# Attention: couplings in quarters spread over the steps, and unread products in TensorE's wait for the second solve

## Chip, core and metric

One core of a Trainium2 chip runs one program of three stages (attention, a Fourier mixer with a feed-forward, a gated spatial unit). The metric is the device time of one execution in microseconds; the engines are TensorE (PE), VectorE (DVE), ScalarE (ACT), GpSimd (POOL), and SyncE (SP), which issues the DMAs.

## What is computed

The change lies in the attention stage, a delta-rule recurrence over 768 tokens for 4 batches of 8 heads (32 heads in all) of width 48:

```python
k_n = k / (np.linalg.norm(k, axis=-1, keepdims=True) + 1e-06)
state = np.zeros((B, H, D, D))
for t in range(S):
    kt, vt, bt = (k_n[:, :, t], v[:, :, t], beta[:, :, t, None])
    y[:, :, t] = np.einsum('bhd,bhde->bhe', q[:, :, t], state)
    v_old = np.einsum('bhde,bhd->bhe', state, kt)
    state = state + bt[:, :, :, None] * np.einsum('bhd,bhe->bhde', kt, vt - v_old)
```

Its result is cast to `[4, 768, 384]` and goes through `_moe_ref` (FFT over tokens and channels, layer norm, two weight products) and `_moe2_ref`; neither is touched but for the counts that they wait for.

## The kernel before

**Tiles.** The tokens are cut into chunks of C = 64. A chunk of one head is solved as a triangular system: with the gram matrix of its keys, the inverse of a unit lower triangular 64x64 matrix is formed, and then the chunk is a handful of small products. There are G = 6 groups; a group holds U = 32 units on each half of the 128 partitions (a unit is a chunk of a head), and is worked off in N = 8 steps of PR = 4 units, so 48 steps. Step k has i = k // 8 (its group) and n = k % 8.

**The inverse.** Each 64x64 inverse is made from its two 32x32 diagonal blocks and a corner. VectorE inverts the diagonal blocks of a whole group at once, 62 dependent column operations (lines 619 and 623) between a transpose in (line 583, `g_lane`, from `g_diag`) and two out (line 630 `t_rows`, line 632 `t_cols`). This is the solve. The corner is -T2 G21 T1, in two rounds of 32-row products on TensorE, the couplings: `couple_w` (line 461, evicted to `w_sb`, line 353) and `couple_x` (line 474, evicted to `tt`, line 361). Before, each of them is done for half a group (HU = 16 units) at a time. `corners` (line 371) spreads `t_cols` over `tt` with two masks. For the last group VectorE, then free, does these evictions (`last_inverse`, lines 655, 661, 666).

**Ahead of the solve** stand `piece("g", g, p)` and `piece("a", g, p)`: a quarter (QU = 8 units) of a group's gram or score products (line 449), 64x64 products, the dense pieces. Gram pieces are made three groups ahead, score pieces one. The couplings and the pieces share two PSUM banks `ps_ga` by turns; `uses` is the list that fixes the order, `turn` the place in it, `ga_done` and `ga_out` count products and evictions. For group 0 the diagonal blocks are copied to `g_diag` by VectorE, ScalarE and GpSimd (lines 638, 380, 309) after all four pieces; for later groups SyncE moves them by DMA.

**A step** on TensorE, in this order: P (line 500, keys by state into `ps_r`), U (line 518, inverse by right-hand side into `ps_u`), for the step before last Y (lines 535 and 540) and S (line 553, state), then pieces and couplings of this step. ScalarE evicts in the same order, each engine waiting by counts, and ScalarE also takes the square root of group i+2's norms in step `ROOT_STEP[i]` (6, 5, 4, 4), which waits for `glane_ok`. In group i before: x of the first half in step 0, w of the second in step 1, x of the second in step 2, w of the next group's first half in step 7; score pieces in steps 2 to 5, gram pieces in 5, 6, 7 and 0.

**Other users.** GpSimd scales v (line 277) and masks scores (line 270), in time with VectorE's columns. SyncE issues loads by the step counts. In the last group the mixer's loads are put into the steps (`ahead`), and its first products behind steps 5 and 6 (line 1110). The mixer starts from the results of the last group's step 4 of `y_sb`.

Of the kernel before, what the change touches and what calls it, by code (L numbers as in the profile page):

```python
# [19 lines left out]
def attention(nc, sems, kq_g, k_g, v_g, beta_g, x_scr):  # L20
# [25 lines left out]
    WARM = 46  # L46
    assert U == 32 and PR == 4 and x_scr.shape[0] == NB
# [3 lines left out]
    uses += [("w", 0, 0), ("x", 0, 0)]  # L51
# [6 lines left out]

    for k in range(STEPS):
        i, n = k // N, k % N  # L60
        if i and n == 0:
            uses += [("x", i, 0)]
        if i and 2 <= n < 6 and i + 1 < G:
            uses += [("a", i + 1, n - 2)]
        if gram_at(i, n):
            uses += [("g",) + gram_at(i, n)]
        if n == 1:
            uses += [("w", i, 1)]
        if n == 2:
            uses += [("x", i, 1)]  # L70
        if n == N - 1 and i + 1 < G:
            uses += [("w", i + 1, 0)]
    turn = {use: m for m, use in enumerate(uses)}

    with ExitStack() as ctx:
# [91 lines left out]
        def coupling(m, rows):  # L167
            return ps_ga[m % 2][rows, 0:HU * H].rearrange("p (u c) -> p u c", c=H)
# [96 lines left out]
        def gpsimd(pool, tokens_clear):  # L265
# [42 lines left out]
            pool.wait_ge(ga_out, turn["g", 0, 3] + 1)  # L308
            pool.tensor_copy(g_diag[quarter(3)], gram_sb[0][quarter(3), 1]).then_inc(dg_pool, 1)
            pool.wait_ge(dg_pool, 1)  # L310
# [11 lines left out]
        def scalar(act):  # L322
# [26 lines left out]
            def solved_w(g, c):  # L349
                m = turn["w", g, c]  # L350
                us = slice(HU * c, HU * c + HU)
                act.wait_ge(ga_done, m + 1)
                act.activation(w_sb[:, us], coupling(m, slice(0, P)), ACT.Copy).then_inc(ga_out, 1)

            def solved_x(g, c):
                m = turn["x", g, c]
                us = slice(HU * c, HU * c + HU)
                act.wait_ge(ga_done, m + 1)
                act.wait_ge(corner_ok, 2 * g + c + 1)
# [4 lines left out]
            def corners(g, c):  # L364

                us = slice(HU * c, HU * c + HU)
# [22 lines left out]
            corners(0, 0)  # L389
            solved_x(0, 0)  # L390
            for k in range(STEPS + 2):
# [11 lines left out]
                if 0 < i < G - 1 and n == 0:  # L403
                    solved_x(i, 0)
# [15 lines left out]
                if i and 2 <= n < 6 and i + 1 < G:  # L420
                    piece("a", i + 1, n - 2)
                if gram_at(i, n):
                    piece("g", *gram_at(i, n))
                if i < G - 1 and n == 1:
                    solved_w(i, 1)
                    corners(i, 1)
                if i < G - 1 and n == 2:
                    solved_x(i, 1)
                if i + 2 < G and n == ROOT_STEP[i]:
                    roots(i + 2)  # L430
                if n == N - 1 and i + 1 < G - 1:
                    solved_w(i + 1, 0)
                    corners(i + 1, 0)

        def tensor(pe, ahead):
# [17 lines left out]
            def couple_w(g, c):  # L453
                m = turn["w", g, c]
# [10 lines left out]
            def couple_x(g, c):  # L465
                m = turn["x", g, c]
# [3 lines left out]
                for j in range(HU):  # L470
                    u = HU * c + j
# [12 lines left out]
            couple_x(0, 0)  # L484
            pe.wait_ge(ident_ok, 2)
            for k in range(STEPS + 2):
# [16 lines left out]
                if 1 <= k <= STEPS:  # L503
                    j0 = k - 1
                    g, m, c = j0 // N, j0 % N, (j0 // NB) % 2
# [15 lines left out]
                if 0 < i < G and n == 0:  # L521
                    couple_x(i, 0)
# [38 lines left out]
                if i and 2 <= n < 6 and i + 1 < G:  # L561
                    piece("a", i + 1, n - 2)
                if gram_at(i, n):
                    piece("g", *gram_at(i, n))
                if n == 1:
                    couple_w(i, 1)
                if n == 2:
                    couple_x(i, 1)
                if n == N - 1 and i + 1 < G:
                    couple_w(i + 1, 0)  # L570

        def vector(dve):
            NEWTON = 5

            def to_lanes(g):
# [3 lines left out]
                else:  # L579
                    dve.wait_ge(dg_dve, 2)  # L580
                    dve.wait_ge(dg_act, 1)
                    dve.wait_ge(dg_pool, 1)
# [43 lines left out]
            def unlanes(g):  # L626
                if g:
                    dve.wait_ge(ga_done, turn["x", g - 1, 1] + 1)
                    dve.wait_ge(corner_ok, 2 * g)
# [6 lines left out]
            dve.wait_ge(ga_out, turn["g", 0, 3] + 1)  # L636
            for a in (0, 2):
                dve.tensor_copy(g_diag[quarter(a)], gram_sb[0][quarter(a), 0]).then_inc(dg_dve, 1)
# [9 lines left out]
            def last_inverse(g):  # L648
# [3 lines left out]
                for c in range(2):  # L652
# [1327 lines left out]
```

## Time and profile before

| what | us |
|---|---|
| median of three runs | 887.49 (886.86 to 890.08) |
| profiled execution, its own time | 889.29 |
| its span, first to last instruction | 887.5 |
| PE busy | 822.8 (93%) |
| DVE busy | 473.3 (53%) |
| ACT busy | 294.3 (33%) |
| POOL busy | 197.8 (22%) |
| attention, up to the results that the mixer needs | 0 to 254.6 |

How to read it: busy shares are means over stages with different limits, so the attention part has to be read by itself. In the timeline and the chain of waits each line has the start, the length and what ran; brackets hold the idle time before it and what ended it; "issue" is time in which the engine waited for nothing that the profile shows. A product of f32 operands shows as two records, so a coupling batch of 32 products has x64.

### The profile page before, as it was taken

Reading aid. Unit: us, or ns where it says so; the run is one execution under the profiler, and the core shown is the slowest. Engines: PE = TensorE matmul, PEld = TensorE weight load, DVE = VectorE, ACT = ScalarE, POOL = GpSimd, SP = SyncE. Lnnn points to the kernel's source line nnn. Section 1 sums busy time; section 2 is a strip of 40 time slices with the busy share of each in tenths; the row PEclk is TensorE's granted clock in tenths of the full one; section 3 lists DMA queues with packets and bytes.
Section 4 is the critical chain, followed back from the end, with each engine's and each line's share of the span. In section 5 each row is a group of like instructions: output and inputs, shape, how many; then the busy total and the mean of one; then the engine's idle time right before and its main releaser. Section 6 shows DMA issues by size and latency. Waiting matters only on the chain.

```text
span 887.5 us, 24710 instructions
## 1 busy us (share of the span) xinstructions
PE 822.8 (93%) x10634; PEld 797.0 (90%) x10634; DVE 473.3 (53%) x1072; ACT 294.3 (33%) x656; POOL 197.8 (22%) x171
## 2 busy tenths in 40 slices
PE   7378999899886999999999999999999999999998
PEld 6377899888776999999999999999899899899898
DVE  4999999999278743443434443333732431431421
ACT  5235566656343121112211221122531431421412
POOL 2123123034005605300720000000222222222321
PEclk9658989889996999999999999999999999999999
DMA  6544445412572120111002003003410010000001
GB/s 196 147 132 125 139 131 155 118 57 80 164 248 96 59 68 18 53 51 40 18 18 71 0 18 119 18 18 112 144 54 31 23 53 35 18 0 36 19 1 54
DMA packets 38170, 65.14 MB, mean 73 GB/s; under 512 B 4345, under 2 KB 26178, under 8 KB 38082
## 3 DMA queue, kind: packets, MB, share of 16 engines
q1 hardware_dynamic: 38082, 63.85, 23.2%
q8 instruction: 69, 1.13, 0.5%
q14 instruction: 19, 0.16, 0.1%
HBM read 46.66 MB, written 14.16 MB: 69 GB/s over the span
## 4 chain that ended last, share of the span: by engine, by line
PE 62%; issue 21%; DVE 13%; POOL 2%; ACT 2%; DMA 1%; SPq 0%; POOLq 0%; DVEq 0%; ACTq 0%
PE m_ps_h L1189 12%; PE g_ps_v L1690 11%; PE m_ps_d L1174 11%; PE ps_ga L449 4%; PE g_ps_y L1690 3%; PE g_ps_u L1690 3%; DVE prod L619 3%; PE ps_r L500 3%; DVE t_lane L623 2%; PE ps_y L540 2%; PE ps_y L535 2%; PE ps_u L518 2%; PE ps_s L553 2%; POOL g_vn_lo L1587 2%; PE ps_ga L474 2%
## 5 line engine op out<-in xcount | busy, mean ns | idle before, releaser
L1374 DVE SCALAR_TENSOR_TENSOR m_h_lo<-m_ps_h,m_h_hi 128x512 fp32r<-128x512 f32 x72 | 49.7, 691 | 101.7 <-ACT m_h_hi L1051 101.7
L1174 PE MATMUL m_ps_d<-m_w_hi,m_h_hi 128*128 128x384 f32 x288 | 97.6, 339 | 0.0
L1174 PE MATMUL m_ps_d<-m_w_hi,m_h_lo 128*128 128x384 f32 x288 | 96.3, 335 | 0.0
L1174 PE MATMUL m_ps_d<-m_w_lo,m_h_hi 128*128 128x384 f32 x288 | 96.3, 334 | 0.0
L1051 ACT ACTIVATE m_h_hi<-m_ps_h 128x512 fp32r<-128x512 f32 x72 | 43.1, 598 | 151.7 <-PE m_ps_h L1189 151.5
L449 PE MATMUL ps_ga<-kq 64*64 64x64 f32 x1536 | 61.0, 236 | 19.0 <-DVE t_lane L623 12.4
L1189 PE MATMUL m_ps_h<-m_unt_hi,m_w_hi 128*128 128x256 f32 x432 | 75.3, 283 | 3.4 <-DVE m_h_lo L1374 2.4
L449 PEld LDWEIGHTS ps_ga<-kq 64*64 64x64 f32 x1536 | 57.3, 150 | 19.9 <-DVE t_lane L623 12.6
L1189 PE MATMUL m_ps_h<-m_unt_hi,m_w_lo 128*128 128x256 f32 x432 | 74.3, 281 | 0.0
L1189 PE MATMUL m_ps_h<-m_unt_lo,m_w_hi 128*128 128x256 f32 x432 | 74.2, 281 | 0.0
L619 DVE TENSOR_TENSOR prod<-g_lane,t_lane 128x31 f32<-128x31 f32 (+15 forms) x186 | 69.6, 374 | 6.2
L623 DVE TENSOR_TENSOR t_lane<-t_lane,prod 128x31 f32<-128x31 f32 (+15 forms) x186 | 66.3, 356 | 6.4
L1851 DVE TENSOR_TENSOR g_vs<-g_ps_v,g_bias 128x384 f32<-128x384 f32 x32 | 17.8, 558 | 92.3 <-PE g_ps_v L1690 92.0
L1587 POOL TENSOR_TENSOR g_vn_lo<-g_vn,g_vn_hi 128x512 fp32r<-128x512 f32 x24 | 30.6, 1288 | 161.3 <-ACT g_vn_hi L1629 161.3
L1189 PEld LDWEIGHTS m_ps_h<-m_unt_hi,m_w_hi 128*128 128x128 f32 x432 | 62.1, 191 | 4.2 <-DVE m_h_lo L1374 2.8
L1690 PE MATMUL g_ps_v<-g_ws_hi,g_vn_hi 128*128 128x384 f32 x192 | 64.4, 335 | 0.0
L1690 PE MATMUL g_ps_v<-g_ws_hi,g_vn_lo 128*128 128x384 f32 x192 | 64.2, 334 | 0.0
L1690 PE MATMUL g_ps_v<-g_ws_lo,g_vn_hi 128*128 128x384 f32 x192 | 64.1, 334 | 0.0
L1593 POOL TENSOR_TENSOR g_g<-g_vs,g_ut 128x384 f32<-128x384 f32 x32 | 36.7, 1147 | 113.9 <-DVE g_vs L1851 113.9
L1189 PEld LDWEIGHTS m_ps_h<-m_unt_hi,m_w_lo 128*128 128x128 f32 x432 | 61.4, 191 | 0.0
L1189 PEld LDWEIGHTS m_ps_h<-m_unt_lo,m_w_hi 128*128 128x128 f32 x432 | 61.4, 191 | 0.0
L540 PE MATMUL ps_y<-u_sb,score 64*64 64x48 f32 x768 | 56.2, 233 | 3.7 <-issue 3.5
(223 smaller groups left out, 1920.7 us busy)
## 6 DMA issues: line engine op xcount, KB each, us to landing
kq<-kq_g SPq DMA_DIRECT2D x48, 256.0 KB, 3.3
v_in<-v_g SPq DMA_DIRECT2D x12, 384.0 KB, 3.3
k_in<-k_g SPq DMA_DIRECT2D x12, 384.0 KB, 3.1
x_scr<-y_sb SPq DMA_DIRECT2D x24, 192.0 KB, 3.5
stage<-w_ch SPq DMA_DIRECT2D x6, 768.0 KB, 5.7
x_scr<-m_x_sb SPq DMA_DIRECT2D x24, 192.0 KB, 1.9
g_x<-x_scr SPq DMA_DIRECT2D x24, 192.0 KB, 4.5
out<-g_y SPq DMA_DIRECT2D x24, 192.0 KB, 1.9
```

The source lines that it names most:

```text
L449: last = pe.matmul(ps_ga[m % 2][lo:lo + C, C * j:C * j + C], x[:, 0], x[:, 0 if what == "g" else 1], start=True, stop=True)
L500: last = pe.matmul(ps_r[lo:lo + C, D * j:D * j + D], kq[i % 4][rows, 0, PR * n + j], s_sb[rows, b, j], start=False, stop=True, skip_group_ ...
L540: last = pe.matmul(ps_y[out, at:at + D], score[g % 2][rows, PR * m + j], u_sb[rows, j0 % 2, j], start=j0 < NB, stop=True)
L619: dve.tensor_tensor(x, g_lane[g % 2][:, j + 1:H, j].unsqueeze(2).broadcast_to([P, m, n]), t_lane[:, j, 0:n].unsqueeze(1).broadcast_to([P, ...
L623: dve.tensor_tensor(below, below, x, ALU.add).then_inc(chain, 1)
L1051: act.activation(h_hi[:, 2 * g:2 * g + 2], ps_h[g % 2][:, :].rearrange("p (f t) -> p f t", f=2), ACT.Relu).then_inc(h_hi_ok, 1)
L1174: last = pe.matmul(out, first[x], second[y], start=(k == 0 and m == 0), stop=(k == n - 1 and m == 2))
L1189: last = pe.matmul(ps_h[g % 2][:, C2 * (f % 2):C2 * (f % 2) + C2], w[:, d, P * f:P * f + P], t[:, d], start=(m == 0 and d == 0), stop=(m = ...
L1374: dve.scalar_tensor_tensor(h_lo[:, 2 * g:2 * g + 2].rearrange("p f t -> p (f t)"), ps_h[g % 2][:, :], 0.0, h_hi[:, 2 * g:2 * g + 2].rearra ...
L1587: pool.tensor_tensor(vn_lo[:, t], vn[:, t % 2], vn_hi[:, t].bitcast(F32), ALU.subtract).then_inc(vn_lo_ok, 1)
L1593: pool.tensor_tensor(g[:, n % 2], vs[:, n % 2], ut[:, f, HS * h:HS * h + HS], ALU.mult).then_inc(g_ok, 1)
L1690: last = pe.matmul(out, first[x], second[w], start=(k == 0 and m == 0), stop=(k == n - 1 and m == 2))
```

## The change

Couplings are done by quarters of a group (q = 0 to 3) and not by halves, and are placed by two functions: w 0 in step 7 of the group before, w 1, 2, 3 in steps 0, 1, 2, x 0 to 3 in steps 0, 2, 4, 6; in the last group earlier. Score pieces move from steps 2 to 5 to steps 1 to 4, so each step of groups 1 and 2 has one dense piece. `couple_x` takes its right operand from `tt` and waits for `corner_ok`, whose count goes from two to three a group. Before the couplings of group 1, TensorE does four products of 512 columns that nobody reads. The first diagonal is copied in three parts. The mixer's waits get the new counts. `ROOT_STEP` stays.

The pieces of the diff are, in order: the placing functions; the first diagonal on ScalarE (VectorE and GpSimd alike); the couplings on TensorE; the wait of the U products of step m; the couplings' places in a step, behind U and at the step's end (ScalarE evicts in the same places); and VectorE's order in the last group.

```diff
+    PARTS = ((1, 0, 16), (2, 16, 24), (3, 24, 32))
...
+    def score_at(i, n):
+        return (i + 1, n - 1) if 1 <= n < 5 and i and i + 1 < G else None
+    def w_at(i, n):
+        if n == N - 1:
+            return [(i + 1, 0)] if i + 1 < G else []
+        if i == G - 1:
+            return {0: [(i, 1)], 1: [(i, 2), (i, 3)]}.get(n, [])
+        return [(i, n + 1)] if n < 3 else []
+    def x_at(i, n):
+        if i == G - 1:
+            return {0: [(i, 0)], 1: [(i, 1)], 2: [(i, 2), (i, 3)]}.get(n, [])
+        return [(i, n // 2)] if n % 2 == 0 else []
...
+        def corner_count(g, q):
+            return 3 * g + min(q, 2) + 1
...
-            for p in range(4):
+            piece("g", 0, 0)
+            for p, u0, u1 in PARTS:
                 piece("g", 0, p)
-            act.wait_ge(ga_out, 4)
-            act.activation(g_diag[quarter(1)], gram_sb[0][quarter(1), 1], ACT.Copy).then_inc(dg_act, 1)
+                act.wait_ge(ga_out, turn["g", 0, p] + 1)
+                act.activation(g_diag[quarter(1), u0:u1], gram_sb[0][quarter(1), 1, u0:u1], ACT.Copy).then_inc(dg_act, 1)
...
+            def keep_warm(m):
+                x = kq[0][:, 0, 0:QU].rearrange("p u t -> p (u t)")
+                for _ in range(4):
+                    pe.matmul(ps_ga[m % 2][0:C, :], x[:, 0:C], x, start=True, stop=True)
+
+            def couple_w(g, q):
+                m = turn["w", g, q]
                 bank_free(m)
+                if (g, q) == (1, 0):
+                    keep_warm(m)
                 pe.wait_ge(trows_ok, g + 1)
-                for j in range(HU):
-                    u = HU * c + j
+                for j in range(QU):
+                    u = QU * q + j
...
+            def couple_x(g, q):
+                m = turn["x", g, q]
                 bank_free(m)
-                pe.wait_ge(tcols_ok, g + 1)
-                pe.wait_ge(ga_out, turn["w", g, c] + 1)
+                pe.wait_ge(corner_ok, corner_count(g, q))
+                pe.wait_ge(ga_out, turn["w", g, q] + 1)
...
-                        last = pe.matmul(coupling(m, upper)[:, j], w_sb[lower, u], t_cols[lower, u],
+                        last = pe.matmul(coupling(m, upper)[:, j], w_sb[lower, u], tt[g % 2][lower, u, H:C],
...
-                    if m % NB == 0:
-                        pe.wait_ge(corner_ok, 2 * g + c + 1)
-                        pe.wait_ge(ga_out, turn["x", g, c] + 1)
+                    if m % 2 == 0:
+                        pe.wait_ge(ga_out, turn["x", g, m // 2] + 1)
+                    if m == 0:
                         pe.wait_ge(v_ok, g + 1)
...
-                if 0 < i < G and n == 0:
-                    couple_x(i, 0)
+                if i < G:
+                    for x in x_at(i, n):
+                        couple_x(*x)
...
-                if i and 2 <= n < 6 and i + 1 < G:
-                    piece("a", i + 1, n - 2)
                 if gram_at(i, n):
                     piece("g", *gram_at(i, n))
-                if n == 1:
-                    couple_w(i, 1)
-                if n == 2:
-                    couple_x(i, 1)
-                if n == N - 1 and i + 1 < G:
-                    couple_w(i + 1, 0)
+                if score_at(i, n):
+                    piece("a", *score_at(i, n))
+                for w in w_at(i, n):
+                    couple_w(*w)
...
+                corners(slice(0, QU))
+                solved_w(0)
+                corners(slice(QU, 2 * QU))
+                corners(slice(2 * QU, U))
+                solved_x(0)
+                solved_w(1)
+                solved_x(1)
+                solved_w(2)
+                solved_w(3)
+                solved_x(2)
+                solved_x(3)
```

## Rows read from the trace of the kernel before

**Rows 1.** Page, part 2: TensorE's granted clock in 40 slices, tenths of full:
```profile
PEclk9658989889996999999999999999999999999999
```

**Rows 2.** TensorE's timeline near 80 us: start, us, instructions, idle before them:
```profile
81.51 1.92 PE L461 MATMUL ps_ga<-t_rows,gram_sb 32*32 32x32 f32 x64 [4.06 <-DVE t_rows L630]
```

**Rows 3.** Windows, groups 1 to 5: from:to, length, then PE, PEld, DVE, ACT, POOL:
```profile
81.50:119.22 37.72, 35.55 (x1153) 34.54 (x1153) 35.21 (x80) 22.30 (x58) 12.30 (x10) 0.87 0.43 123
119.22:155.76 36.54, 34.11 (x1155) 33.20 (x1153) 34.00 (x79) 23.29 (x59) 8.96 (x7) 0.91 0.49 140
155.76:191.73 35.97, 32.93 (x1058) 31.84 (x1056) 33.54 (x76) 21.51 (x55) 8.69 (x6) 0.86 0.34 94
191.73:225.49 33.76, 29.82 (x1028) 28.62 (x1025) 28.75 (x62) 20.76 (x54) 9.23 (x6) 0.95 0.28 81
225.49:254.60 29.11, 25.29 (x814) 23.88 (x813) 15.57 (x23) 11.83 (x36) 0.50 (x2) 0.94 0.62 195
```

**Rows 4.** VectorE's timeline: the transposes to t_rows of groups 1 to 5:
```profile
79.34 2.02 DVE L630 STREAM_TRANSPOSE t_rows<-t_lane 128x1024 f32<-128x1024 f32 x1
...
113.20 2.12 DVE L630 STREAM_TRANSPOSE t_rows<-t_lane 128x1024 f32<-128x1024 f32 x1
...
147.22 2.14 DVE L630 STREAM_TRANSPOSE t_rows<-t_lane 128x1024 f32<-128x1024 f32 x1
...
182.86 2.12 DVE L630 STREAM_TRANSPOSE t_rows<-t_lane 128x1024 f32<-128x1024 f32 x1
...
216.56 2.11 DVE L630 STREAM_TRANSPOSE t_rows<-t_lane 128x1024 f32<-128x1024 f32 x1
```

**Rows 5.** Windows along the granted clock, TensorE alone: from:to, length, busy, clock:
```profile
47.10:67.60 20.50, 17.71 (x437) 0.50 0.38 122
...
67.60:81.20 13.60, 9.64 (x325) 1.00 0.62 182
...
81.20:91.50 10.30, 9.99 (x250) 0.50 0.07 23
...
122.20:129.00 6.80, 6.80 (x166) 0.50 0.10 36
...
159.70:166.50 6.80, 6.15 (x135) 0.50 0.21 57
...
231.40:234.80 3.40, 3.40 (x76) 0.50 0.37 113
```

**Rows 6.** Chain of waits, 145 to 260 us: start, us, what:
```profile
168.19 1.13 PE ps_ga L461 x64
...
169.32 0.60 PE ps_r L500 x16
...
228.25 1.43 issue
...
250.60 0.83 PE m_ps_o L1110 x4
...
251.43 0.65 PE m_ps_e L1110 x4
```

**Rows 7.** Timelines of VectorE and ScalarE at the start:
```profile
11.67 2.13 DVE L638 COPY g_diag<-gram_sb 32x1024 f32<-32x1024 f32 x2 [9.65 <-ACT gram_sb L342]
...
13.85 1.28 ACT L335 ACT_TABLE_LOAD   x1
...
15.82 0.35 ACT L335 ACTIVATE root<-g_lane,tiny 128x32 f32<-128x32 f32 x1 [0.68 <-DVE g_lane L583]
```

**Rows 8.** Timelines of ScalarE and VectorE: square roots, and a transpose:
```profile
75.08 0.36 ACT L335 ACTIVATE root<-g_lane,tiny 128x32 f32<-128x32 f32 x1 [0.60 <-DVE g_lane L583]
...
140.92 2.00 DVE L583 STREAM_TRANSPOSE g_lane<-g_diag 128x1024 f32<-128x1024 f32 x1
...
144.77 0.34 ACT L335 ACTIVATE root<-g_lane,tiny 128x32 f32<-128x32 f32 x1
```

**Rows 9.** GpSimd's timeline: the scaling of v for group 4:
```profile
176.71 2.77 POOL L277 TENSOR_TENSOR v_in<-v_in,norm 128x1536 f32<-128x1536 f32 x1 [23.18 <-DMA v_in<-v_g]
```

More of the change, by code:

```diff
@@ L362, in solved_x, with corners @@
                 last.then_inc(ga_out, 1)
-            def corners(g, c):
-                us = slice(HU * c, HU * c + HU)
+            def corners(g, us):
                 act.wait_ge(tcols_ok, g + 1)
@@ L388, in scalar @@
             solved_w(0, 0)
-            corners(0, 0)
-            solved_x(0, 0)
+            corners(0, slice(0, QU))
             for k in range(STEPS + 2):
@@ L402, in scalar @@
                     preset(k + 1)
-                if 0 < i < G - 1 and n == 0:
-                    solved_x(i, 0)
+                if i < G - 1:
+                    for x in x_at(i, n):
+                        solved_x(*x)
                 if k >= 2:
@@ L419, in scalar @@
                     continue
-                if i and 2 <= n < 6 and i + 1 < G:
-                    piece("a", i + 1, n - 2)
                 if gram_at(i, n):
                     piece("g", *gram_at(i, n))
+                if score_at(i, n):
+                    piece("a", *score_at(i, n))
+                for g, q in w_at(i, n):
+                    if g < G - 1:
+                        solved_w(g, q)
                 if i < G - 1 and n == 1:
[L425 to L428, printed above, removed]
+                    corners(i, slice(QU, 2 * QU))
+                if i < G - 1 and n == 3:
+                    corners(i, slice(2 * QU, U))
                 if i + 2 < G and n == ROOT_STEP[i]:
@@ L431, in scalar @@
                 if n == N - 1 and i + 1 < G - 1:
-                    solved_w(i + 1, 0)
-                    corners(i + 1, 0)
+                    corners(i + 1, slice(0, QU))
         def tensor(pe, ahead):
@@ L635, in vector @@
                 dve.memset(t[:, :], 0.0).then_inc(s_zero, 1)
-            dve.wait_ge(ga_out, turn["g", 0, 3] + 1)
-            for a in (0, 2):
-                dve.tensor_copy(g_diag[quarter(a)], gram_sb[0][quarter(a), 0]).then_inc(dg_dve, 1)
+            for p, u0, u1 in PARTS:
+                dve.wait_ge(ga_out, turn["g", 0, p] + 1)
+                for a in (0, 2):
+                    dve.tensor_copy(g_diag[quarter(a), u0:u1], gram_sb[0][quarter(a), 0, u0:u1]).then_inc(dg_dve, 1)
             to_lanes(0)
@@ L651, in last_inverse, with corners @@
                 dve.wait_ge(u_done, N * (g - 1))
-                for c in range(2):
-                    us = slice(HU * c, HU * c + HU)
+                def corners(us):
                     for a in range(2):
@@ L657, in last_inverse, with solved_w, solved_x @@
                     part.then_inc(corner_ok, 1)
-                    m = turn["w", g, c]
+                def solved_w(q):
+                    m = turn["w", g, q]
                     dve.wait_ge(ga_done, m + 1)
                     dve.wait_ge(ga_out, m)
-                    dve.tensor_copy(w_sb[:, us], coupling(m, slice(0, P))).then_inc(ga_out, 1)
-                    m = turn["x", g, c]
+                    dve.tensor_copy(w_sb[:, QU * q:QU * q + QU], coupling(m, slice(0, P))).then_inc(ga_out, 1)
+                def solved_x(q):
+                    m = turn["x", g, q]
                     dve.wait_ge(ga_done, m + 1)
-                    dve.wait_ge(corner_ok, 2 * g + c + 1)
+                    dve.wait_ge(corner_ok, corner_count(g, q))
                     for a in (0, 2):
-                        part = dve.tensor_scalar(tt[g % 2][quarter(a), us, H:C], coupling(m, quarter(a)), -1.0, None,
-                                                 ALU.mult)
+                        part = dve.tensor_scalar(tt[g % 2][quarter(a), QU * q:QU * q + QU, H:C], coupling(m, quarter(a)),
+                                                 -1.0, None, ALU.mult)
                     part.then_inc(ga_out, 1)
+                corners(slice(0, QU))
[9 more added lines that the diff above has]
+                solved_x(3)
             last_inverse(G - 1)
         done = {"y_done": y_done, "s_done": s_done, "u_done": u_done, "y_ok": y_ok, "s_ok": s_ok, "states": STEPS - NB, "y_out": y_out, "ga_out": ga_out,
-                "ga_done": ga_done, "corner_ok": corner_ok, "pieces": len(uses), "steps": STEPS, "groups": G, "n": N}
+                "ga_done": ga_done, "corner_ok": corner_ok, "pieces": len(uses), "w_last": turn["w", G - 1, 3] + 1, "corners": 3 * G, "steps": STEPS, "groups": G, "n": N}
         return (sync, gpsimd, scalar, tensor, vector), done
@@ L1082, in scalar @@
             act.wait_ge(att["ga_done"], att["pieces"])
-            act.wait_ge(att["corner_ok"], 2 * last_group + 2)
+            act.wait_ge(att["corner_ok"], att["corners"])
             act.wait_ge(w_lo, DT - 1)
@@ L1254, in first_weights_split @@
                 dve.wait_ge(att["ga_done"], att["pieces"])
-                dve.wait_ge(att["corner_ok"], 2 * last_group + 2)
+                dve.wait_ge(att["corner_ok"], att["corners"])
                 for c in range(DT - 1):
```

66 lines of the change are left out of this document (28 added, 38 removed).

## The prediction

> **What bounds the kernel now.** First view: the granted clock in forty slices [rows 1]. It reads 8 or less in six of the first ten slices, which are the attention part, and 9 in all behind the thirteenth. Second: TensorE's wait for the second solve [rows 2]: its first coupling batch of group 1 starts at 81.51 after 4.06 us of idle that VectorE's t_rows ended. Until there VectorE sets the pace, and everything that shifts VectorE's start shifts 81.51. Third: TensorE's work by group [rows 3]. The five stretches start where the first coupling batch of groups 1 to 5 starts; the last ends at the y_sb on which the mixer waits. TensorE is busy 94, 93, 92, 88 and 87% of them, so it bounds this part. Fourth: when the solves end [rows 4]. t_rows is ready at 81.36, 115.32, 149.36, 184.98 and 218.67. TensorE asks for it at 81.51, 119.22, 155.76, 191.73 and 225.49: from the second on VectorE is 3.9, 6.4, 6.8 and 6.8 us ahead. That lead is all that a faster TensorE can win before VectorE bounds. Fifth: TensorE's clock [rows 5]. It stands at 0.50 (1.2 GHz) for 20.5 us from 47.1, for 10.3 from 81.2, for 6.8 from 122.2 and again from 159.7, and for 3.4 us each in three more stretches, of which the one at 231.4 stands for the others (in groups 3 and 4).
>
> **Price of the low clock.** A coupling batch of 64 takes 1.92 us at 1.2 GHz [rows 2] and 1.13 at 2.4 [rows 6]: factor 1.70. A busy microsecond at the low clock thus gives back 0.4. Busy time at the low clock [rows 5]: group 1, 10.0 (worth 4.0); group 2, 6.8 (2.7); group 3, 6.2 and 3.4 (3.8); groups 4 and 5, 3.4 each (1.4 each). Sum 13.3 us. Without it the groups would last 33.7, 33.8, 32.2, 32.4 and 27.7 us [rows 3].
>
> **Part 1, the first diagonal copied in three parts.** Before, VectorE starts two copies of 32x1024 only after the last gram piece, 2.13 us from 11.67; ScalarE loads its square-root table at 13.85 after copy and scores, and starts the root at 15.82, 0.68 after it was free, when the transpose ended [rows 7]. After, only the last quarter is left behind the last piece: VectorE 2.13/4, or about 0.6 with the fixed cost, so the transpose could start 1.3 us sooner. ScalarE then becomes the later one: of its copy a quarter is left, so its table is ready about 0.7 sooner, plus the 0.68 that it had to spare, less small waits between the parts. I take **0.9 us** (bounds 0.5 and 1.4) for root, chain and t_rows alike: the second solve ends at 80.46.
>
> **Part 2, group 0 under the second solve.** Its couplings start in quarters, so the first u step needs 0.96 us of products twice instead of 1.92 twice, and short evictions: about 1.6 us sooner, on top of the 0.9. This is not on the path. ScalarE's square root for group 2 stands in step 6, waits for VectorE's transpose already now (0.60 idle, root at 75.08 [rows 8]) and will do so 0.9 earlier. The last piece of group 0 then ends near 76.5 (before it ended at 81.51 - 4.06 = 77.45).
>
> **Part 3, the four unread products** (64 rows out, 512 columns, K of 128). No such row exists. Nearest: two products of 193 columns in 0.83 us, and the next two in 0.65 [rows 6]. By columns one of 512 costs 0.86 to 1.10, four 3.4 to 4.4 us; I take 3.9. They run from 76.5 to 80.4 against t_rows at 80.46: hidden, and at most 0.5 too long. Behind them in TensorE's queue stands the whole of group 1. What they bring is the clock: group 1 starts at 2.4 GHz, which is worth **4.0 us** (bounds 0 and 4.0).
>
> **Part 4, quarters and one dense piece to a step.** The number of coupling products stays, 4.5 us a group; a step loses either a second dense piece (step 5) or gets its missing one (step 1). TensorE's busy time is unchanged. Evictions are more and shorter (for x two of 32x256 instead of 32x512, with no drop in fixed cost, so some 0.4 us more of ScalarE a group): hidden, ScalarE is busy 22.30 of 37.72 us [rows 3]. x now waits for corner_ok instead of tcols_ok, that is, for a ScalarE eviction; it has the P products (0.60 us [rows 6]) and the U products, as many, as cover, about what w and corners of a quarter take. What is to be won is the clock of groups 2 to 5: all low stretches there begin in steps 0 to 2, where the full coupling batches (32-row products) stand beside a halt of about 1 us in instruction issue, as the 1.43 us at 228.25 [rows 6]. With half the couplings there and a dense piece in each step I expect most of the **9.3 us** to go; I keep one or two short stretches (bounds 0 and 9.3).
>
> **What is late next.** Two things cut the gain. (a) ScalarE's root for group i+2 keeps its place in step 4 or 5. In group 2 it ran at 144.77, behind a transpose that ended at 142.92 [rows 8]. Transpose minus 0.9 is 142.0; TensorE, 4.7 us ahead at the start (114.5 for 119.22) and 2.7 more without the low clock, would bring ScalarE there at 137.4. It stalls 4.6 us; TensorE can run one step further (about 1.8), so **2.8 us** are lost, and perhaps 1.4 with a clock that falls in this wait. (b) VectorE itself: t_rows 5 at 218.67 - 0.9 = 217.8; the interval before group 4 was 35.62 instead of 34 because GpSimd's v_in waited for its DMA until 176.71 [rows 9] and its 2.77 us then fell beside column steps; with loads issued sooner this 1.6 goes, so 216.15 is the **floor** for group 5.
>
> **The sum.** Group 1 starts at 80.6, ends at 114.3; group 2 may start at 114.5 (t_rows), 33.8 + 2.8 + 1.4 gives 152.5; + 32.2 = 184.7; + 32.4 = 217.1 for the start of group 5, before 225.49. In group 5 VectorE evicts: t_cols, corners of a quarter and w come 3 us after t_rows, so x starts near 219.2 and not at 218.9 (217.1 + 1.8 for the w products, P and U): + 0.3. Then 27.7: y_sb at 245.1 instead of 254.6, **9.5 us** saved. One short low stretch more in groups 3 to 5, 1.4 us: 8.1. The mixer's front is fed by that y_sb; its loads are tied to the same steps and shift along, nothing is added. The profiled execution has a span of 887.5 and a time of 889.29; 889.29 - 8.1 = 881.2. It lay 1.8 us over the median 887.49 of the three runs, which carries over: **879.5**.
>
> **Rivals.**
> A, the forecast: 0.65. Own range 875.5 (floor reached, no low stretch, 12 us) to 882.5.
> B, spreading doesn't hold the clock: the fall comes from a pause of the engine, not from what the products are. Then only the fall after the 4.06 us wait goes, 0.9 + 4.0 = 4.9 us, and 882.6 results; root and t_rows bind nowhere, since the lead is only 3.9 + 4.0. For it: the longest low stretch in the groups stands behind the only long wait. Against it: the stretch from 47.1 stays at 0.50 while TensorE is busy 17.7 of 20.5 us [rows 5], and the later falls have pauses of some 1 us, such as also stand in full-speed stretches. 0.20. The Trainium skill, "TensorE: Matmul & The Clock Gate", section "HAM oscillation — how this bites in real kernels", ties the fall to the engine's idle gaps between bursts; by that rule B is the outcome, and the busy but slow stretch from 47.1 speaks against it.
> C, the fill-in work doesn't carry the clock (it runs at 1.2 GHz and the rise comes later, or root's wait of group 0 lets it fall) and spreading helps little: 0.9 to 4 us, 883.5 to 886.6. 0.09.
> D, slower: the small couplings in steps 4 and 6 of group 0 keep it at 1.2 GHz up to the unread products. The last three steps (9.6 busy us in 13.6, now at 2.4 [rows 5]) then take 6.4 longer, the unread products up to twice 3.9 (less as the clock rises in them); from 77.45 - 2.5 that makes a start of group 1 near 88, 6.7 late, minus the 4.0 that its warm clock gives. With one low stretch more in each of four groups, 1.4 each, from the couplings in steps 4 and 6: +8.3, 895.8. It decides from the point where the unread products end later than 85.5. 0.06. Against it: the root of group 0 leaves TensorE time, and no start of group 1 is bound by it before.
>
> **How the numbers follow.** B's centre lies on the limit, so 0.6 of it counts as faster. Faster by over 0.5% (below 883.05; 0.5% is about what a measurement of this kernel can tell from no change): 0.65 + 0.13 = 0.78; same 0.17; slower 0.05. The range takes A and nearly all of B: 875.5 to 884.5.
>
> **What would show it.** Root of group 0 at 14.9. t_rows 1 near 80.5 and TensorE's wait before it about 0, with the clock at 1.00 until well behind 90. Four f32 products of 512 columns in 3.4 to 4.4 us. Clock near 1.00 in groups 2 to 5. In group 2 ScalarE waits for g_lane before the root. Group 5 starts at 216 to 218.5. Wrong would be: low stretches as before (B), unread products that end behind t_rows by microseconds (D), or an interval from group 5's start to y_sb over 31 us.

## The result and the profile after

The changed kernel takes 898.81 us (median; 895.77 to 902.07) where the kernel before takes 887.8 beside it: ratio 1.0121, 95% interval 1.0077 to 1.0164. It is slower by some 11 us, where 8 us of gain were forecast. The profiled execution has a span of 898.5 us and a time of 900.24, against 887.5 and 889.29 of before.

The granted clock in forty slices; [rows 1] answers to it. The slices about group 1 are now 9, and group 5 (the eleventh and twelfth) has fallen to 6 and 8:
```profile
PEclk9659999999686899999999999999999999999999
```

The windows of groups 1 to 5, columns as in [rows 3], which answer to them:
```profile
81.60:118.05 36.45, 32.94 (x1153) 31.22 (x1152) 33.94 (x80) 23.78 (x66) 10.90 (x9) 1.00 0.45 126
118.05:157.40 39.35, 32.91 (x1156) 31.25 (x1155) 36.50 (x88) 24.38 (x68) 9.04 (x7) 1.00 0.47 131
157.40:193.80 36.40, 32.10 (x1061) 30.31 (x1062) 33.84 (x76) 22.94 (x63) 8.72 (x6) 0.95 0.33 92
193.80:226.30 32.50, 29.34 (x1026) 27.56 (x1028) 25.31 (x52) 21.81 (x62) 9.12 (x6) 1.00 0.29 87
226.30:259.50 33.20, 32.13 (x813) 30.65 (x813) 15.32 (x31) 11.82 (x36) 0.50 (x2) 0.69 0.50 158
```
Read the third and the last but two columns together. In groups 1 to 4 the clock is 1.00, 1.00, 0.95, 1.00 where it was 0.87, 0.91, 0.86, 0.95, and TensorE is busy 5.1 us less in them. But the groups last 144.7 us where they lasted 144.0: the idle time, length minus busy, went from 11.6 to 17.4. Group 5 lasts 33.2 for 29.1 at a clock of 0.69.

The windows along the granted clock, TensorE alone, columns as in [rows 5]:
```profile
45.60:69.50 23.90, 20.70 (x469) 0.50 0.42 127
69.50:81.60 12.10, 11.89 (x300) 1.00 0.54 160
230.00:250.50 20.50, 20.43 (x476) 0.50 0.34 109
294.80:301.60 6.80, 5.53 (x26) 0.50 0.00 0
```

**The ledger.** From the start of group 1 to the y_sb that the mixer waits for, the length can be split in three: TensorE's busy time as it would be at 2.4 GHz (the busy time less 0.41 of what lay in stretches at 0.50; 0.41 is 1 - 1/1.70, the factor of the prediction), the price of the low clock (that 0.41), and idle time. This was done for all kernels, each by its windows. Column "G1, G2-5" is the time at 0.50 in group 1 and in groups 2 to 5. The mixer takes its batches in turns; a turn is counted from the start of the second piece of ScalarE's m_unt_hi (277.93 and 306.50 in before, 284.85 and 317.78 in after), and "front" goes from that y_sb to the second turn. Behind it, each of these executions took 580.7 to 581.0 us.

| kernel | couplings | full-speed work | low price | idle | length | at 0.50: G1, G2-5 | front |
|---|---|---|---|---|---|---|---|
| before | halves | 144.1 | 13.6 | 15.4 | 173.1 | 9.9, 23.9 | 51.9 |
| after | quarters | 149.7 | 9.8 | 18.5 | 177.9 | 0, 23.9 | 58.3 |
| e1, changed again | quarters | 148.5 | 11.2 | 16.3 | 175.9 | 3.4, 23.9 | 57.9 |
| e2 | halves | 144.0 | 10.5 | 14.5 | 169.0 | 0, 27.3 | 50.9 |
| e4 | quarters | 148.2 | 11.2 | 14.0 | 173.4 | 3.4, 23.9 | 57.6 |
| e5 | quarters | 147.9 | 13.9 | 14.7 | 176.4 | 3.4, 30.7 | 52.4 |
| e6 | halves | 144.4 | 13.4 | 16.8 | 174.7 | 9.2, 23.9 | 51.3 |
| e7 | quarters, last group halves | 148.8 | 10.7 | 15.4 | 175.0 | 3.4, 23.9 | 50.4 |
| e8 | halves | 143.4 | 13.9 | 15.8 | 173.1 | 3.4, 30.7 | 53.3 |
| e9 | quarters | 148.0 | 19.4 | 13.0 | 180.4 | 17.0, 30.7 | 57.4 |
| e10 | quarters | 148.6 | 16.7 | 15.8 | 181.1 | 6.8, 34.2 | 58.2 |
| e11 | halves | 143.4 | 13.6 | 15.5 | 172.5 | 3.4, 30.7 | 52.9 |

From before to after: work +5.6, low price -3.8, idle +3.1, start of group 1 +0.1, front +6.4. That is 11.4, and the spans differ by 11.0: 0.3 less lies behind the second turn, the rest is rounding. Each row is one execution, and executions of one kernel lie up to 13 us apart (e1: 892.91 to 906.11; e2's profiled one, 884.5 us, is its fastest of ten). So a column is read over several rows, and a time is taken from the medians.

Two places of the trace of after carry the terms. TensorE's timeline at the start of group 1:
```profile
78.01 3.65 PE L476 MATMUL ps_ga<-kq 128*64 128x512 f32 x8
81.59 0.60 PE L488 MATMUL ps_ga<-t_rows,gram_sb 32*32 32x32 f32 x26
```
The unread products (L476) take 3.65 us and end 1.4 behind t_rows, which is ready at 80.24; before, [rows 2] had 4.06 us of idle here.

TensorE's and ScalarE's timelines in group 1, step 4:
```profile
102.00 0.68 PE L545 MATMUL ps_u<-r_sb,tt 64*64 64x48 f32 x16
103.72 0.69 PE L502 MATMUL ps_ga<-tt,w_sb 32*32 32x32 f32 x32 [1.05 <-issue]
...
102.31 1.32 ACT L387 ACTIVATE tt<-t_cols,half 128x512 f32<-128x512 f32 x2
103.53 0.32 ACT L411 ACTIVATE r_sb<-ps_r 128x192 f32<-128x192 f32 x1
```
ScalarE's corners (L387) end at 103.63; x (L502), which now waits for corner_ok, starts 0.09 later after 1.05 us of idle. "issue" hides this: the releaser is a count. It stands so in step 4 of groups 1 to 3 (1.05, 1.05 and 1.03 us) and with 0.59 in group 4. R's eviction (L411) stands behind the corners as well.

### The profile page after: what moved, and what is told of

Its sections match the earlier page's. It is cut to its first block, busy times and chain, and to the rows that moved or that the text cites. A ratio compares the mean times of both kernels' runs of the same rounds, so it can differ in the third digit from the quotient of the medians.

```text
span 898.5 us, 24817 instructions
## 1 busy us (share of the span) xinstructions
PE 832.1 (93%) x10642; PEld 800.1 (89%) x10642; DVE 474.2 (53%) x1084; ACT 301.0 (34%) x698; POOL 199.0 (22%) x173
## 4 chain that ended last, share of the span: by engine, by line
PE 65%; issue 21%; DVE 8%; POOL 2%; ACT 2%; DMA 1%; SPq 0%; POOLq 0%; ACTq 0%; DVEq 0%
PE m_ps_h L1230 12%; PE m_ps_d L1215 11%; PE g_ps_v L1731 11%; PE ps_ga L467 4%; PE g_ps_y L1731 3%; PE ps_y L563 3%; PE ps_r L527 3%; PE ps_y L568 3%; PE ps_u L545 3%; PE ps_ga L502 2%; PE ps_s L581 2%; POOL g_vn_lo L1628 2%; PE g_ps_u L1731 2%; PE ps_ga L488 2%; DVE m_w_lo L1311 2%
## 5 line engine op out<-in xcount | busy, mean ns | idle before, releaser
L467 PE MATMUL ps_ga<-kq 64*64 64x64 f32 x1536 | 58.7, 229 | 21.0 <-DVE t_lane L647 12.4
L643 DVE TENSOR_TENSOR prod<-g_lane,t_lane 128x31 f32<-128x31 f32 (+15 forms) x186 | 72.0, 387 | 6.2
L467 PEld LDWEIGHTS ps_ga<-kq 64*64 64x64 f32 x1536 | 54.4, 144 | 21.6 <-DVE t_lane L647 12.6
L647 DVE TENSOR_TENSOR t_lane<-t_lane,prod 128x31 f32<-128x31 f32 (+15 forms) x186 | 63.8, 343 | 6.4
L1040 POOL TENSOR_TENSOR m_u<-m_x_tok,m_pmq 128x193 f32<-128x193 f32 x12 | 7.1, 592 | 233.6 <-DVE m_ppq L1353 176.4
```

The costliest lines, as they stand in the source:

```text
L467: last = pe.matmul(ps_ga[m % 2][lo:lo + C, C * j:C * j + C], x[:, 0], x[:, 0 if what == "g" else 1], start=True, stop=True)
L643: dve.tensor_tensor(x, g_lane[g % 2][:, j + 1:H, j].unsqueeze(2).broadcast_to([P, m, n]), t_lane[:, j, 0:n].unsqueeze(1).broadcast_to([P, ...
L647: dve.tensor_tensor(below, below, x, ALU.add).then_inc(chain, 1)
```

## The experiments

All were timed beside the kernel before: e1 to e4 together (before 889.85 us), e5 to e8 (890.37), e9 to e11 (891.23).

### e1: the changed kernel again

> The changed kernel once more, as the base of the three runs beside it. If the 898.8 us were a matter of the chip or of the phase in which TensorE's clock happens to fall, this profile should show other low stretches and a time that may lie near 890. If they are of the kernel, group 5 again stands at 1.2 GHz for most of its first 20 us (229.7 to 250.2 in the profiled run), groups 1 to 4 again run at 2.4 GHz and still take 36.5, 39.4, 36.4 and 32.5 us, and the time is 896 to 902.

Measured: 898.66 us, ratio 1.0089 (1.0043 to 1.0134). The loss stands, and is the yardstick of e3 and e4. Group 5 again stands at 0.50, for 17.1 us; but groups 1, 2 and 4 have 3.4 us each of it, where the expectation had full clock, and last 37.1, 38.1 and 32.3 us.

### e2: only the unread products

```diff
+                if (g, c) == (1, 0):
+                    keep_warm(m)
                 pe.wait_ge(trows_ok, g + 1)
```

> The kernel before with the four unread products alone. Theory 1 (a busy microsecond at 1.2 GHz costs 0.4 us, as the prediction had it, and the gain was lost elsewhere): group 1 lasts about 34 us instead of 37.7, its busy time falls from 35.6 to 31.5, and the time is 3 to 4 us under before. Theory 2 (the clock is worth half of that, since the couplings alone scale by 1.7 and the rest by less): busy time 33 to 33.5, 1 to 2 us under before. The end of the unread products decides too: behind t_rows (81.36) by up to 1 us costs that much.

Measured: 890.4 us, ratio 0.9991 (0.9954 to 1.0029). Its windows of groups 1, 2 and 5:
```profile
81.70:115.80 34.10, 31.76 (x1153) 30.50 (x1152) 31.73 (x74) 22.54 (x59) 8.80 (x7) 1.00 0.49 135
115.80:153.20 37.40, 34.67 (x1154) 33.63 (x1154) 34.89 (x80) 23.23 (x59) 11.77 (x10) 0.91 0.49 139
220.90:250.70 29.80, 26.17 (x814) 24.89 (x812) 15.70 (x24) 11.77 (x36) 0.50 (x2) 0.89 0.63 196
```
Group 1 lasts 34.1 us at full clock, where the prediction had 33.7. So the price of 0.4 per busy microsecond holds, with couplings in halves. This is also the row against which the quarters can be read: group 1 of after has the same clock (1.00) and the same count of instructions (1153), and takes 36.45 us, 1.2 busy and 1.2 idle us more. Group 2 says the same at clock 1.00: TensorE is busy 32.9 us in after and 31.8 in e6, whose couplings are in halves. The groups of instructions of L488 and L502 in group 1 of after, then of the same products (L468 and L481) in e2, by busy time and mean ns:
```profile
L488 PE MATMUL ps_ga<-t_rows,gram_sb 32*32 32x32 f32 x128 | 3.0, 193 | 0.0
L502 PE MATMUL ps_ga<-tt,w_sb 32*32 32x32 f32 x128 | 2.8, 192 | 1.5 <-issue 1.5
```
```profile
L468 PE MATMUL ps_ga<-t_rows,gram_sb 32*32 32x32 f32 x128 | 2.6, 192 | 0.4 <-issue 0.4
L481 PE MATMUL ps_ga<-t_cols,w_sb 32*32 32x32 f32 x128 | 2.4, 192 | 0.0
```
The same 256 records cover 5.8 us in eight batches and 5.0 in four: 0.8 of the 1.2. In time, e2 is no faster than before within 0.4%, though its profiled execution is; the 3 to 4 us that the expectation had under theory 1 did not come.

### e3: the last group's couplings in halves again

```diff
-            return [(i + 1, 0)] if i + 1 < G else []
+            return [(i + 1, q) for q in range(2 if i + 1 == G - 1 else 1)] if i + 1 < G else []
...
-            return {0: [(i, 0)], 1: [(i, 1)], 2: [(i, 2), (i, 3)]}.get(n, [])
+            return {0: [(i, 0), (i, 1)], 2: [(i, 2), (i, 3)]}.get(n, [])
```
Besides, w 1 goes from step 0 to the step before, and VectorE's corners and evictions stand in the same order.

> The changed kernel, but the couplings of the last group stand as before: two quarters of w back to back in the step before it, both x in step 0, the other w in step 1, x in step 2, VectorE evicting in that order. Theory 1 (cutting the last group's couplings into a chain TensorE, VectorE, TensorE in steps 0 to 2 without any dense piece is what lets the clock fall): group 5 up to its y_sb takes 28 to 30 us instead of 33.2, the time is 4 to 8 us under the changed kernel. Theory 2 (the fall comes from a halt in instruction issue that happens to lie there): group 5 stays at 32 to 34 us.

Measured: 894.55 us, ratio 1.0034 (0.9991 to 1.0077), 4.1 below e1, with intervals that overlap. Its profiled execution is its slowest (902.31 us) and stands in no table. Group 5 lasted 29.9 us in it (231.24 to 261.1), with 10.2 at 0.50, against 33.2 and 33.1 in after and e1. Group 1 starts at full clock in it and then has some 10 us at 0.50, from 94.4 on.

### e4: the corners ahead of ScalarE's wait for the state

ScalarE makes the corners of steps 1, 3 and 7 (in step 7 from group 2 on) before it waits for S of the step, and no longer behind y and the score. The code below is that of step 3.
```diff
+                if i < G - 1 and n == 3:
+                    corners(i, slice(2 * QU, U))
...
-                if i < G - 1 and n == 3:
-                    corners(i, slice(2 * QU, U))
```

> The changed kernel, but ScalarE's corners stand ahead of its wait for S in steps 1, 3 and 7 (in step 7 from group 2 on), so that x does not wait for them. Theory 1 (x waits on ScalarE's corners): the 1.05 us of idle before x of step 4 (102.68, 141.17, 180.44, and 0.59 at 213.14) and the 0.25 us before other x go, in sum 5 us in groups 1 to 4, and the start of group 5 moves from 226.3 to 221 to 222. Theory 2 (the idle is instruction issue): it stays. In the time it shows in full unless VectorE's solve for group 5 (217.5) or the last group's clock takes it.

Measured: 893.4 us, ratio 1.0026 (0.9995 to 1.0057), 5.3 below e1, with intervals that overlap a little; it is clear of the first reading of the changed kernel (1.0077 to 1.0164). TensorE's waits between 81 and 260 us by line, the sum, how many and the longest: x in after (L502), then in e4 (L504):
```profile
PE ps_ga L502 <- issue: 7.5, 13, 1.5
```
```profile
PE ps_ga L504 <- issue: 2.7, 4, 1.0
```
Before had 2.9 in 3 waits at this place. The wait for the corners is real: one of 1.03 to 1.05 us stands in step 4 of group after group in all six profiled executions of quarters with late corners, and in neither e4 nor e7. In after the waits of this kind add up to some 5 us. As a sum over the row, x waits 5.0 to 7.5 us with late corners and 2.7 and 3.9 with early ones, so 3 to 5 us is what the edit gives. They go when the corners are made while ScalarE stands idle.

### e5 and e6: GpSimd's first fold behind VectorE's first weight halves

In the mixer's front GpSimd's first fold (L880 and L878 in after: sum and difference of halves of its input, 128x1536) runs beside VectorE's low halves of the weights (m_w_lo, 128x1536). The same wait was added to the changed kernel (e5) and to the kernel before (e6). It adds no work.
```diff
+            pool.wait_ge(w_lo, DT + 2)
             fold_in(0)
```

> The changed kernel; in the mixer GpSimd's fold of batch 1 waits until VectorE has done the two low weight halves that stand behind the first turn. Theory 1 (of the 11 us that the second batch's turn is late, some 4.5 arise there, because GpSimd's fold starts 0.8 us ahead of these two operations and holds VectorE for 9.2 us, where before it started 1.6 us behind them and held it 6.7): the two take 3.4 to 3.6 us, and the distance from the y_sb that the mixer waits for to the second turn falls from 58 to 52 us; the time is 4 to 6 us under the changed kernel. Theory 2 (the front is late because of TensorE's low clock there, not of VectorE): the two operations get shorter, the distance stays above 56.

> The same wait in the kernel before. By theory 1 it gains less than in the changed kernel: the two operations fall from 6.7 to 3.5 us, 2 to 3 us under before, and the spread of its executions (886 to 899) narrows if the race between the two engines makes part of it. By theory 2 nothing changes; and if GpSimd's later fold is missed by the next batch's spectrum, it gets slower by up to 2 us.

Measured: e5 894.29 us, ratio 1.0044 (1.0016 to 1.0072); e6 889.53, ratio 0.9994 (0.9965 to 1.0022). The wait seems to give 4 us to the changed kernel (the interval of e5 overlaps that of e1, but not that of the first reading) and nothing that can be measured to the one before. Timelines of VectorE and GpSimd in the mixer's front, of before, of after and of e5:
```profile
279.28 6.72 DVE L1270 TENSOR_TENSOR m_w_lo<-stage,m_w_hi 128x1536 fp32r<-128x1536 f32 x2
280.84 3.55 POOL L839 TENSOR_TENSOR m_half<-m_x_in_sb 128x1536 f32<-128x1536 f32 x1 [2.33 <-issue]
284.34 5.01 POOL L837 TENSOR_TENSOR m_x_in_sb<-m_x_in_sb 128x1536 f32<-128x1536 f32 x1
```
```profile
286.19 9.22 DVE L1311 TENSOR_TENSOR m_w_lo<-stage,m_w_hi 128x1536 fp32r<-128x1536 f32 x2
295.34 1.28 DVE L1415 SCALAR_TENSOR_TENSOR m_h_lo<-m_ps_h,m_h_hi 128x512 fp32r<-128x512 f32 x2
...
285.39 3.47 POOL L880 TENSOR_TENSOR m_half<-m_x_in_sb 128x1536 f32<-128x1536 f32 x1
288.83 4.97 POOL L878 TENSOR_TENSOR m_x_in_sb<-m_x_in_sb 128x1536 f32<-128x1536 f32 x1
```
```profile
284.80 3.42 DVE L1312 TENSOR_TENSOR m_w_lo<-stage,m_w_hi 128x1536 fp32r<-128x1536 f32 x2
...
288.35 3.50 POOL L880 TENSOR_TENSOR m_half<-m_x_in_sb 128x1536 f32<-128x1536 f32 x1 [4.32 <-DVE m_w_lo L1312]
291.81 3.50 POOL L878 TENSOR_TENSOR m_x_in_sb<-m_x_in_sb 128x1536 f32<-128x1536 f32 x1
```
Alone, VectorE's pair takes 3.42 and each fold of GpSimd 3.50. Together they take turns, one instruction at a time. In after GpSimd is 0.80 ahead: VectorE's first waits until 288.86, runs 1.7, its second waits until GpSimd's second has run, and m_h_lo, for which TensorE waits, comes 5.8 us late. In before VectorE is 1.56 ahead, gets its first through, and loses 3.3. In e5 nothing collides. From the first turn to the second the front takes 28.6 us in before, 32.9 in after, 27.8 in e5, 27.7 in e6. This holds over the rows: with quarters and without the wait GpSimd is ahead in all six executions, and the stretch takes 31.3 to 33.6 us; with quarters and the wait (e5, e7) it takes 27.8 twice; with halves and without it, 27.5 to 28.6.

### e7: corners early, last group in halves, and the fold's wait

> The changed kernel with the three repairs at once: corners early, last group's couplings in halves, GpSimd's fold waiting. If x waiting for corners (5 us), the low clock of group 5 (4 us) and the fold (5 us) are separate causes, 14 us go and it lies at 884 to 886, under before; if they share a cause, or VectorE's solve stops the gain, it stays at 888 to 892.

Measured: 890.07 us, ratio 0.9982 (0.9952 to 1.0012). The second case of the expectation came: with the three repairs the changed kernel is back at the time of before, not below it. This interval is clear of both readings of the changed kernel, so the three together do remove the loss. Group 1 is at full clock but for 3.4 us, and in this execution the work of the quarters (148.8 for 144.1) eats that.

### e8 and e11: only the first diagonal in parts and three unread products, in the kernel before

e8 has the fold's wait as well, e11 doesn't.
```diff
+    PARTS = ((1, 0, 16), (2, 16, 24), (3, 24, 32))
...
+                for _ in range(3):
+                    pe.matmul(ps_ga[m % 2][0:C, :], x[:, 0:C], x, start=True, stop=True)
...
+                if (g, c) == (1, 0):
+                    keep_warm(m)
```

> The kernel before with the first diagonal in three parts, three unread products and GpSimd's fold waiting; the couplings stay in halves. If quartering is what eats the gain (group 1 at full clock 34.1 us in halves, 36.5 in quarters), this lies under before by 0.9 + 3 + 2.5, at 883 to 885. If the gain of the full clock in group 1 is lost further on whatever the couplings (VectorE's solve ends at 114.5 and 148.5, ScalarE's root waits for it), it lies at 886 to 888.

> The kernel before with two parts of the change alone, the first diagonal in three parts and three unread products, and without the wait that holds GpSimd's first fold behind VectorE's first weight halves (the same kernel with that wait: 888.35, ratio 0.9965). Theory: the wait pays only where GpSimd would start ahead of VectorE. In the two kernels with couplings in halves whose front was seen, VectorE was ahead by 1.6 and 1.7 us, so here it is too, and the time is the same within 1 us. Rival: the wait was worth the 4.4 us that it was worth in the changed kernel, and this one is at 890 to 893.

Measured: e8 888.35 us, ratio 0.9965 (0.9934 to 0.9997); e11 888.72, ratio 0.9982 (0.9950 to 1.0013). These two parts of the change, with the wait, have the lowest ratio of this study, 0.35% below before, with an interval that just leaves 1 out and overlaps that of e7: that halves beat the repaired quarters is not shown in time. The 883 to 885 us of the expectation did not come. With three products group 1 starts at 80.77, 0.06 behind t_rows (80.71), and at full clock. But the full clock of group 1 did not stay a gain: from there to y_sb both executions have 34.1 us at 0.50 in all, and before has 33.8. In e11 the fold started 1.09 us behind VectorE's pair, which took 6.70 us, so the collision was there in the mild form of before. From turn to turn the front takes 28.5 us in e11 and 27.7 in e8; the times can't tell the two apart, as expected.

### e9: the changed kernel without the unread products

> The changed kernel without the four products that nobody reads; all else as changed. Prediction's theory (the unread products buy group 1's full clock, 4.0 us by 0.4 a busy us, and cost the 1.3 us by which they ended behind t_rows): group 1 starts near 80.3, stands at 0.50 for about 10 us, lasts about 40.5 us where it lasted 36.5 and 37.1, and the time is 2 to 3 us above 898.7 as measured beside the other runs of the changed kernel. Rival (the low clock is only moved: the stretch that is bought off in group 1 comes back in another group, as the totals of 24 to 34 us at 0.50 between the start of group 1 and y_sb in all kernels so far suggest): the total at 0.50 stays between 24 and 34 us, and the time is within 1.5 us of 898.7, or lower.

Measured: 901.48 us, ratio 1.0128 (1.0097 to 1.0160). Its window of group 1:
```profile
80.20:120.80 40.60, 39.07 (x1154) 37.90 (x1154) 37.85 (x87) 24.11 (x66) 12.49 (x10) 0.79 0.40 116
```
Group 1 starts 1.4 us sooner, 0.15 behind t_rows, at 0.50 for its first 13.6 us, and lasts 40.6 us where it lasted 36.45 and 37.1. The total at 0.50 is 47.7 us, outside the 24 to 34 to which the rival had bound it. So the products do buy group 1's clock, about 4 us for 1.4. The rival isn't dead for that: in halves the total is 33.8 and 33.0 us without the products and 27.3, 34.1 and 34.1 with them, and none of e2, e8 and e11 shows the 4 us in its time. In time this one lies 2.8 us above e1, as forecast, but the ratios (1.0128 against 1.0121 and 1.0089) overlap.

### e10: the score pieces back in steps 2 to 5

```diff
-        return (i + 1, n - 1) if 1 <= n < 5 and i and i + 1 < G else None
+        return (i + 1, n - 2) if 2 <= n < 6 and i and i + 1 < G else None
```

> The changed kernel with the score pieces back in steps 2 to 5, so that step 1 has couplings and no dense piece and step 5 two dense pieces. Prediction's theory (a dense piece in each step holds the clock): without it the clock of groups 1 and 2 falls in steps 0 to 2 again, 6.8 us at 0.50 each, 2.7 us each: about 904. Theory now (the place of a dense piece carries nothing): 898.7 give or take 1.5, the total at 0.50 from group 1 to y_sb between 24 and 34 us as in all others.

Measured: 901.61 us, ratio 1.0114 (1.0080 to 1.0149), between the two readings of the changed kernel. Its windows of groups 1 and 2:
```profile
81.70:121.70 40.00, 35.77 (x1153) 34.20 (x1152) 37.18 (x89) 23.97 (x66) 11.05 (x9) 0.91 0.42 117
121.70:161.90 40.20, 36.82 (x1154) 35.33 (x1152) 37.43 (x85) 24.38 (x68) 8.79 (x6) 0.87 0.44 126
```
6.8 and 10.2 us at 0.50 look like the prediction's theory. But e5 and e7, with a dense piece in every step, also have 10.2 us in group 2. The other side missed too: the total at 0.50 is 41.0 us, outside its 24 to 34. On the clock this run settles nothing by itself. It does settle one thing: the full-speed work stays at 148.6 us with the score pieces where they were, so their move isn't what added work.

## Why the prediction was wrong, point by point

In short: the forecast was 8 us of gain, nearly all of it clock. Group 1's clock came, that of groups 2 to 5 did not, and three costs that stood at nothing came on top: some 5 us of TensorE work in the quarters, x's waits for ScalarE's corners, and a collision of VectorE and GpSimd in the mixer.

**Part 1** was right. The root of group 0 starts at 14.62 (forecast 14.9), and t_rows of group 1 is ready at 80.24 for 81.36 [rows 4], 1.1 us sooner for 0.9. **Part 2**: the last piece of group 0 ended at 78.08, not 76.5, as the low stretch from 45.6 lasted 23.9 us for 20.5.

**Part 3.** The size was right (3.65 for 3.9, bounds 3.4 to 4.4), and so was what it buys: clock 1.00 in group 1. The start has the best support of all: in the nine executions of the table with unread products, and in e3's, group 1 starts at full clock, in the three without it starts at 0.50. How much is won is less sure: the nine have 0 to 6.8 us at 0.50 in group 1, the three 9.2 to 17.0, but e3's slowest execution has some 10 as well. "Hidden, and at most 0.5 too long" was wrong: they began 1.5 us late, and so ended 1.4 behind t_rows. Three of them fit (e8).

**Part 4 is the step that failed**, in four of its sentences.

"TensorE's busy time is unchanged": the instructions are, the time they cover isn't. Full-speed work is 143.4 to 144.4 us in five executions with couplings in halves, 147.9 to 149.7 in seven with quarters (e7's last group apart). This is the mis-sized term: 0 where it was about 5 us. It lies in the quarters by exclusion: halves with the unread products (e2), and with the diagonal in parts as well (e8, e11), don't have it, quarters without the products (e9) or with the score pieces back (e10) do. From group 1 to 5 there are 20 more coupling batches, so an estimate from these numbers is 0.25 us a batch. The rows of e2 and after give 0.8 of 1.2 us in group 1 to the coupling batches themselves; where the rest lies isn't shown.

"It has the P products and the U products as cover": it has, if ScalarE comes to the corners in time. ScalarE made them behind S, y and score of the step before, and 1.32 us of corners started when P had begun. I had looked at ScalarE's share of the stretch (22.30 of 37.72 us), not at what stands ahead of the corners in its order. In after these waits add up to some 5 us, and e4 removes them. ScalarE's own extra work was mis-sized as well, 1.0 to 1.5 us a group for 0.4 (22.30 to 23.78 in group 1), but that is hidden.

"I expect most of the 9.3 us to go": none went. Groups 2 to 5 have 23.9 us at 0.50 before and 23.9 after; over all quarter kernels 23.9 to 34.2, over all with halves 23.9 to 30.7. Of the clock only what rival B had given was gained, group 1. That the low stretches begin in steps 0 to 2 was seen rightly; that spreading the couplings would remove them wasn't borne out.

And group 5: the stretches didn't vanish but gathered. It stands at 0.50 for 20.5 us, with TensorE busy 20.43 of them. In five of six executions with quarters in the last group it is 17.1 to 20.5 us, in the sixth (e5) 0; with halves 3.4 to 13.7. It lasts 33.2 us, over the 31 that the prediction had named as a sign of being wrong. The Trainium skill, "TensorE: Matmul & The Clock Gate", section "HAM oscillation — how this bites in real kernels", puts such a fall down to idle gaps of the engine. The start of group 1 agrees (4.06 us of wait and a fall, or filled and none). This stretch agrees less: at its start stands a wait of 1.07 us, but waits of 1.05 and 1.53 us in groups 1 and 2 of the same trace had no fall behind them, and inside it there are no gaps.

**What is late next.** (a) The stall is there, but small. In after ScalarE's root in group 2 (145.82) waited for nothing, and in e2 it waited 1.2 us for VectorE, not 4.6. In e2 group 2 started at 115.8, 1.3 later than forecast, and had 6.8 us at 0.50, worth 2.7. (b) The floor never bound: group 5 started at 226.3.

**The mixer**: "its loads are tied to the same steps and shift along, nothing is added". 6.4 us were added, the largest single term. 4.4 of them lie between the two turns, where GpSimd's fold collides with VectorE's weight halves; e5 removes the collision, the stretch falls from 32.9 to 27.8 us, and the time is 4.4 us below e1. Part of the stretch is the clock that falls along with it: 0.80 in after, 0.92 in before, 0.88 in e5. Who comes first changed sides by 2.4 us of relative timing: from VectorE 1.56 ahead to GpSimd 0.80 ahead. The first 2.0 us lie ahead of the first turn. There SyncE issued the two big stage loads at 247.57 (before 241.16), closer to the y_sb that must go out, and that transfer took 4.94 us for 3.22. That the one caused the other was argued only; no run separated it. And over the rows the way from y_sb to the first turn takes 23.3 to 25.6 us with halves and 22.7 to 26.4 with quarters, so these 2.0 us can't be laid to the change.

**The rivals.** B had the clock right and the sign wrong. D, the slower one, gave 895.8, near the result, by another road: the unread products ended at 81.66, not behind its 85.5, and the losses came from work, corners and mixer. No rival had a price for quartering itself, which is where every bound of "0 and 9.3" should have reached below nothing.

Open are why the low stretches in groups 2 to 5 come where they come, why group 5 of e5 has none, and whether the full clock bought in group 1 is paid back behind it. Why GpSimd comes first in the front of every quarter kernel without the wait wasn't looked into either.

## What to carry to other kernels

Cutting a batch of small products in two isn't free though its instructions are the same: here each half became two quarters that together cover 0.2 us more (5.8 us for 5.0 over four halves), and it drags more borders and waits in; price it from a border in the trace. Before an operation gets a new wait, read what stands ahead of the releasing instruction on its own engine, not how busy that engine is. A shift of a few microseconds can turn round which of two engines comes first at a place far behind the edit, so look there for pairs whose length depends on the order, and fix the order with a wait.

## What the runs showed of the hardware

In these traces large elementwise instructions of VectorE and GpSimd, with both operands in SBUF, exclude each other: 128x1536 f32 takes 1.7 us on VectorE and 3.5 on GpSimd, and when both are ready the one waits for the other's whole instruction (pairs of 3.42, 6.7 and 9.2 us by who came first). The Trainium skill, "Trainium Architecture — The Big Picture", section "What this means for kernel authors", says that the port pair of the two engines is taken under an exclusive lock; the three timelines agree.

TensorE at work isn't enough for its clock: 20.43 busy of 20.50 us at 1.2 GHz in group 5, 39.07 busy of 40.60 at a mean clock of 0.79 in group 1 of e9. And a wait of 2.5 us (e9) was followed by 13.6 us at 0.50, waits of 3.6 and 4.1 us (e6, before) by 9.2 and 9.95, while with the wait filled by products of 512 columns and 64 rows out the clock was 1.00 on the far side, in ten executions of ten.
